# The last ten pairs of a convolution and two MLPs on one core, in an order of their own

## What is computed

```python
def _moe_ref(x, w_in, w_out):
    h = x @ w_in
    g = np.maximum(0.01 * h, h)
    return g @ w_out

def _moe2_ref(x, w_in, w_out, a, b):
    h = x @ w_in
    h2 = h * h
    h3 = h2 * h
    P = a[0] + a[1] * h + a[2] * h2 + a[3] * h3
    Q = 1.0 + np.abs(b[0]) * np.abs(h) + np.abs(b[1]) * h2
    g = P / (Q + 1e-06)
    return g @ w_out
```

## Time and profile before

| | us |
|---|---|
| median of 3 runs | 1347.91 (1347.9 to 1348.41) |
| the profiled execution | 1347.41 |
| its span, first to last instruction | 1345.5 |
| busy in the span: TensorE | 1264.7 (94%) |
| VectorE | 1059.5 (79%) |
| ScalarE | 1033.0 (77%) |
| GpSimd | 618.7 (46%) |

### The profile page before, as it was taken

The page is one execution under the profiler, slowest core; times in us unless marked ns, Lnnn a source line. Parts: engine busy times, 40 slices in busy tenths (PEclk is TensorE's granted clock), DMA queues, the critical chain, the costliest instruction groups (busy, mean ns, idle before and its releaser), DMA issues.

```text
span 1345.5 us, 14840 instructions
## 1 busy us (share of the span) xinstructions
PE 1264.7 (94%) x5724; PEld 1027.6 (76%) x5724; DVE 1059.5 (79%) x945; ACT 1033.0 (77%) x1027; POOL 618.7 (46%) x265
## 2 busy tenths in 40 slices
PE   7989999999999999999999999999999999999774
PEld 6768787877878787787877878787787878778553
DVE  3667878878788788878878787877878788787896
ACT  4677777878777877887877877787787788788763
POOL 0034454544545445445445454454544544545664
PEclk8999999999999999999999999999999999999887
DMA  6200000000000000000000000000000000000000
GB/s 191 78 1 13 0 25 1 12 13 1 24 1 25 0 12 13 1 25 0 13 13 13 13 0 25 1 12 14 12 13 1 25 1 13 1 1 12 0 12 12
DMA packets 25093, 21.74 MB, mean 16 GB/s; under 512 B 2909, under 2 KB 23997, under 8 KB 25023
## 3 DMA queue, kind: packets, MB, share of 16 engines
q1 hardware_dynamic: 25023, 20.80, 5.3%
...
## 4 chain that ended last, share of the span: by engine, by line
PE 58%; DVE 20%; ACT 11%; POOL 5%; issue 4%; DMA 1%; POOLq 0%; SPq 0%; DVEq 0%; ACTq 0%
PE h L611 29%; DVE den L508 6%; PE acc L621 5%; PE acc L630 5%; PE acc L631 5%; PE acc L623 5%; PE acc L622 5%; DVE hi L496 5%; DVE den L502 5%; POOL den L313 4%; ACT rec L394 4%; ACT rec L397 2%; ACT hi L389 2%; ACT h L385 2%; PE h L576 2%
## 5 line engine op out<-in xcount | busy, mean ns | idle before, releaser
L313 POOL TENSOR_TENSOR den<-den,rec 128x1024 f32<-128x1024 f32 x128 | 313.2, 2447 | 706.3 <-DVE den L508 415.6
L611 PE MATMUL h<-xs,wa 128*128 128x512 f32 x2520 | 612.5, 395 | 25.3 <-DVE xs L475 15.0
L611 PEld LDWEIGHTS h<-xs,wa 128*128 128x128 f32 x2520 | 471.5, 189 | 145.5 <-DVE xs L475 19.9
L319 POOL TENSOR_TENSOR lo<-den,rec 128x1024 fp32r<-128x1024 f32 x128 | 308.6, 2411 | 11.0 <-DVE den L508 11.0
L496 DVE SCALAR_TENSOR_TENSOR hi<-pol,coef_a,rec 128x1024 fp32r<-128x1024 f32 x128 | 164.3, 1283 | 94.6 <-issue 48.3
L621 PE MATMUL acc<-hi,wb 128*128 128x512 f32 x512 | 206.4, 403 | 20.0 <-DVE xs L489 19.9
L522 DVE TENSOR_TENSOR lo<-h,hi 128x1024 fp32r<-128x1024 f32 x128 | 156.3, 1221 | 86.8 <-ACT hi L389 86.8
L630 PE MATMUL acc<-lo,wb 128*128 128x512 f32 x512 | 201.5, 394 | 20.1 <-POOL lo L319 20.1
L363 ACT ACTIVATE rec<-h 128x1024 f32<-128x1024 f32 x124 | 127.3, 1027 | 111.6 <-PE h L611 111.6
L385 ACT ACTIVATE h<-h 128x1024 f32<-128x1024 f32 x128 | 129.3, 1010 | 98.6 <-PE h L611 98.6
L623 PE MATMUL acc<-hi,wb 128*128 128x512 f32 x512 | 201.0, 393 | 0.0
...
## 6 DMA issues: line engine op xcount, KB each, us to landing
...
```

The lines of the kernel that those rows point to most:

```text
L313: nc.gpsimd.tensor_tensor(den[k][:, :], den[k][:, :], rec[n % RECS][:, :], ALU.mult).then_inc(s_den, 1)
L319: nc.gpsimd.tensor_tensor(lo2[k][:, :], den[k][:, :], rec[(n - 1) % RECS][:, :], ALU.mult).then_inc(s_lo2, 1)
L611: last = T.matmul(dst[:, half, :], lhs, xs[m][:, part, :], start=(j == 0), stop=(j == 4))
```

## The change

Pairs 118 to 127 get a function of their own, `tail(n)`, on TensorE, ScalarE, VectorE and GpSimd; the steps before them stay as they were. In it:
- the hidden tiles go through three PSUM tensors by a table, `tail_ps`: 118 `h2`, 119 `h1`, 120 `acc0`, 121 `h2`, 122 `h1`, 123 `acc0`, 124 `h1`, 125 `acc0`, 126 `h2`, 127 `h1`;
- the third power of the polynomial is written in place in PSUM (`pol_3_all`), and `quotient_hi` and `residue` read it there. A hidden tile is therefore in use until the residue, where before it was free after the polynomial, and the up matmuls of a later pair wait for `s_res` instead of `s_pol`;
- the denominator has three buffers, `den0`, `pol1` and `den1`, and the polynomial's first power only `pol0`;
- ScalarE does the reciprocal of pair n-1 behind the first three instructions of pair n, VectorE the quotient of pair n-1 behind the polynomial of pair n, GpSimd the low part of pair n-2 behind the denominator of pair n, and TensorE the down matmuls of pair n-3 behind the up matmuls of pair n (`LAG2_TAIL = 3`);
- block 14 leaves at n = 123 (moves) and 124 (transposes into `h2`, copies); the last block's transposes go into `acc0`.

```diff
+LAG2_TAIL = 3
+TAIL_FOLD, TAIL_OUT, TAIL_END = 5, 6, 3
...
+    TAIL = PAIRS - LEAD
...
+        tail_ps = (h2, h1, acc[0], h2, h1, acc[0], h1, acc[0], h2, h1)
+
         def hidden_2(n):
 
-            if n > PAIRS - LEAD and n % 2:
-                return acc[0] if n > PAIRS - STEPS else h1
-            return h2
+            return tail_ps[n - TAIL] if n >= TAIL else h2
+
+        def den_of(n):
+
+            return (den[0], pol[1], den[1])[(n - TAIL) % 3] if n >= TAIL else den[n % 2]
+
+        def pol_of(n):
+
+            return pol[0] if n >= TAIL else pol[n % 2]
+
+        def pol_3_all(n):
+
+            return hidden_2_all(n) if n >= TAIL else pol[n % 2][:, :]
...
+            # GpSimd
+            def tail(n):
+                if n < PAIRS:
+                    denominator(n)
+                if n == TAIL:
+                    quotient_lo(TAIL - 1)
+                if TAIL <= n - 2 < PAIRS:
+                    quotient_lo(n - 2)
...
+            # ScalarE
+            def tail(n):
+                if n == TAIL + 1:
+                    split_x2(BLOCKS - 1)
+                if n < PAIRS:
+                    absolute(n)
+                    slope(n)
+                    first_power(n)
+                if n == TAIL + TAIL_FOLD:
+                    out_leaves(BLOCKS - 2)
+                if n == TAIL + TAIL_OUT:
+                    out_copies(BLOCKS - 2)
+                if TAIL <= n - 1 < PAIRS:
+                    reciprocal(n - 1)
+                if n == PAIRS + TAIL_END:
+                    out_leaves(BLOCKS - 1)
+                    out_copies(BLOCKS - 1)
...
             # VectorE
             def quotient_hi(n):
...
-                V.scalar_tensor_tensor(hi2[k][:, :], pol[k][:, :], coef_a[:, 0:1], rec[n % RECS][:, :],
+                V.scalar_tensor_tensor(hi2[k][:, :], pol_3_all(n), coef_a[:, 0:1], rec[n % RECS][:, :],
...
-                V.scalar_tensor_tensor(pol[k][:, :], pol[k][:, :], coef_a[:, 1:2], hidden_2_all(n),
+                V.scalar_tensor_tensor(pol_3_all(n), pol_of(n)[:, :], coef_a[:, 1:2], hidden_2_all(n),
...
+            def tail(n):
+                if n == TAIL + 1:
+                    split_x2(BLOCKS - 1)
+                if n == TAIL + TAIL_OUT:
+                    out_sums(BLOCKS - 2)
+                if n < PAIRS:
+                    polynomial(n)
+                if n == TAIL + TAIL_FOLD:
+                    out_moves(BLOCKS - 2)
+                if TAIL <= n - 1 < PAIRS:
+                    quotient_hi(n - 1)
+                    product(n - 1)
+                    residue(n - 1)
...
+            # TensorE
+            def tail(n):
+                c = BLOCKS - 1
+                if n == TAIL + TAIL_OUT:
+                    pe.wait_ge(s_res, n - 2)
+                    transpose_out(c - 1)
+                if n < PAIRS:
+                    if n == TAIL:
+                        pe.wait_ge(s_pol, n)
+                    elif n == TAIL + 1:
+                        pe.wait_ge(s_lo1, PAIRS)
+                    elif n == TAIL + 2:
+                        pe.wait_ge(s_x2_lo, 2 * c + 1)
+                    elif n == TAIL + 8:
+                        pe.wait_ge(s_ot_sum, 2 * c)
+                    else:
+                        pe.wait_ge(s_res, n - 1 if n > TAIL + 5 and n < TAIL + 8 else n - 2)
...
+                    up(1, n, hidden_2(n), x2_rest_ready, s_h2)
+                k0 = n - LAG2 if n < TAIL + LAG2 else n - LAG2_TAIL
+                if n != TAIL + LAG2 and k0 < PAIRS:
...
+                    pe.wait_ge(s_hi2, k0 + 1)
+                    down(1, k0, hi2[k], lo2[k], lambda: pe.wait_ge(s_lo2, k0 + 1), s_acc2)
```

More of the change, by code:

```diff
@@ L187, in runs, with every_step @@
             return 0 <= index < count
-        def every_step(step):
-            for n in range(-LEAD, PAIRS + OUT_AT + 1):
+        def every_step(step, tail):
+            for n in range(-LEAD, TAIL):
                 step(n)
+            for n in range(TAIL, PAIRS + TAIL_END + 1):
+                tail(n)
         order = [0, 1, 4, 2, 3, 5, 6, 7] + list(range(PIECES, 2 * PIECES))
@@ L345, in _, with absolute, slope, first_power @@
             nc.scalar.preload_act_table(ACT.Abs_reciprocal_sqrt)
+            def absolute(n):
+                if n == 0:
+                    act.wait_ge(s_coef, 2)
+                    act.wait_ge(s_wlo, 2 * PIECES)
+                act.wait_ge(s_h2, n + 1)
+                wait(act, s_lo2, n + 1 - RECS)
+                nc.scalar.activation(rec[n % RECS][:, :], hidden_2_all(n), ACT.Abs).then_inc(s_abs, 1)
+            def slope(n):
+                act.wait_ge(s_abs, n + 1)
+                if n == TAIL + 1:
+                    act.wait_ge(s_res, TAIL)
+                else:
+                    wait(act, s_lo2, n - 2 if n > TAIL + 2 else TAIL if n == TAIL + 2 else n - 1)
+                nc.scalar.activation(den_of(n)[:, :], rec[n % RECS][:, :], ACT.Identity, scale=coef_b[:, 1:2],
+                                     bias=coef_b[:, 0:1]).then_inc(s_slope, 1)
+            def first_power(n):
+                if n > TAIL:
+                    act.wait_ge(s_pol, n)
+                wait(act, s_res, min(n, TAIL) - 1)
+                nc.scalar.activation(pol_of(n)[:, :], hidden_2_all(n), ACT.Identity, scale=coef_a[:, 3:4],
+                                     bias=coef_a[:, 2:3]).then_inc(s_lin, 1)
+            def reciprocal(n):
+                r = rec[n % RECS][:, :]
+                act.wait_ge(s_den, n + 1)
+                nc.scalar.activation(r, den_of(n)[:, :], ACT.Abs_reciprocal_sqrt,
+                                     bias=one[:, 0:1]).then_inc(s_rsq, 1)
+                act.wait_ge(s_rsq, n + 1)
+                nc.scalar.activation(r, r, ACT.Square).then_inc(s_rec, 1)
+            def split_x2(c):
+                act.wait_ge(s_acc1, STEPS * c + STEPS)
+                wait(act, s_h2, STEPS * c)
+                nc.scalar.activation(xs[1][:, 0:3:2, :], acc[0][:, :, :], ACT.Copy).then_inc(s_x2_hi, 1)
+            def out_copies(c):
+                act.wait_ge(s_ot, c + 1)
+                wait(act, s_stored, 16 * c)
+                for half in range(2):
+                    nc.scalar.activation(out_tok[:, 2 * half:2 * half + 2, :], out_half(c, half)[:, :, 0:D],
+                                         ACT.Copy).then_inc(s_ot_copy, 1)
             def step(n):
@@ L366, in step @@
                 if phase == OUT_AT and runs(o0, BLOCKS):
[L367 to L376 removed]
+                    out_copies(o0)
@@ L398, in step @@
+                act.wait_ge(s_lky, m0 + 1)
+                wait(act, s_acc1, m0 - 1)
+                nc.scalar.activation(hi1[m0 % 2][:, :], hidden_1_all(n), ACT.Copy).then_inc(s_hi1, 1)
+                for j in range(*split_with(m0)):
+                    split_hi(j)
+                if n >= 0:
+                    reciprocal(n)
                 if phase == FOLD_AT and runs(o0, BLOCKS):
                     out_leaves(o0)
+            def tail(n):
+                if n == TAIL + 1:
+                    split_x2(BLOCKS - 1)
+                if n < PAIRS:
+                    absolute(n)
+                    slope(n)
+                    first_power(n)
+                if n == TAIL + TAIL_FOLD:
[7 more added lines that the diff above has]
+                    out_copies(BLOCKS - 1)
@@ L416, in _ @@
             split_hi(2)
-            every_step(step)
+            every_step(step, tail)
         @block.vector
@@ L533, in out_sums @@
                     rest = out_tok[:, 2 * half:2 * half + 2, P:D]
-                    V.tensor_tensor(rest, out_half(half)[:, :, D:2 * P], rest, ALU.add).then_inc(s_ot_sum, 1)
+                    V.tensor_tensor(rest, out_half(c, half)[:, :, D:2 * P], rest, ALU.add).then_inc(s_ot_sum, 1)
             def step(n):
```

122 lines of the change are left out of this document (50 added, 72 removed).

## The result

| | before | after |
|---|---|---|
| median, us | 1348.11 (4 runs, 1347.9 to 1348.41) | 1358.96 (4 runs, 1357.86 to 1360.31) |
| profiled span, us | 1345.5 | 1357.1 |

The changed kernel takes 1.0081 of the time before, with a 95% interval of 1.0063 to 1.0098: slower by 11 us.

What follows compares the result with a forecast made beforehand. The tail, through VectorE and GpSimd, was taken to bound the kernel. Long waits of 18.8 us less a gain of 8.4 gave +10.4, so 1358.3 us; 8 in 10 within 1352.5 to 1362.5.

Steps and rivals of the forecast that it cites:

- What it removes: Tail: VectorE no longer collides with GpSimd on SBUF ports (12 us); a late pair costs 7.14 us instead of 8.36.
- the ring: Late tail: loop of absolute, slope, denominator and low part through rec and GpSimd, 7.14 us per pair.
- Pair 118: Tail start: reciprocal now behind ScalarE's split and three instructions of the next pair; residue 118 ends 6.3 us late.
- Pairs 120 to 122: Up of 121 waits for residue 118, down of 120 for the move-out of acc1; residue 122 ends 3.3 us late.
- Pairs 123 and 124: Ups of 124 and 125 wait for residues 122 and 123: steps of 13.3 and 14.4 us, residue 124 14.3 late.
- The end: Pairs 125 to 127: two loops of 7.14, then 4.9 us with product blocked 1.0; residue 127 ends 10.4 late.
- three rings: Long waits at pairs 122 to 124, adding 5.3 + 6.2 + 7.3 = 18.8 us over steps of 7.14.
- The closing stretch: From the last residue to the span's end: 11.45 us, the same work in both kernels, so 0 change.
- A: Rival: the tail's rings don't close, only the 7.14 us loop is left, a gain, 1339.5 us; 4%.
- B: Rival: TensorE's three bursts after gaps of 6 to 9 us run at 2.4 GHz, 5 us less, 1353.3; 12%.
- C: Rival: PSUM operands don't free the port, pairs step at 8.36 as before, 1366 us; 6%.
- D: Rival: overlapping handovers make the waits cost less than half, within 0.2% of before, 1348 us; 5%.

Runs made afterwards that it cites:

- e10: e5 with the polynomial kept in SBUF instead of in place in PSUM; 1348.52 us, 1.0009 of before.
- e5: Changed kernel with the one-pair lag undone, down matmuls two pairs behind and block 14's sums moved out at n = 121; 1337.34 us, 0.9929 of before.
- e4: Changed kernel with the polynomial kept in SBUF and a new third denominator buffer; 1367.83 us, 1.0153 of before.
- e7: e3 with a fourth buffer for rec, so absolute of pair n waits for the low part of n-4; 1338.24 us, 0.9928 of before.
- e1: Changed kernel with block 14's sums moved out of acc1 ahead of pair 123's polynomial and ScalarE instructions; 1353.94 us, 1.0046 of before.
- e2: Changed kernel with h2, h1, acc0 used in turn and block 14 transposed into h1 at n = 128; 1344.26 us, 0.9974 of before.
- e6: Changed kernel with 16 unread matmuls added before the up of 125, where TensorE was idle; 1355.58 us, 1.0060 of before.
- e0: The changed kernel run again, unedited, as yardstick; 1358.83 us, 1.0085 of before.
- e3: Changed kernel with the edits of e1 and e2 together; 1340.70 us, 0.9950 of before.

## Why the prediction was right

**What it removes.** Right. The place of the polynomial was the cause of the blocked time (e10 against e5: 11 us; e4, with a wait of its own in it: 9), and all residues fell to 1.28 us. The section on the cores says that the engines meet only at semaphores; VectorE and GpSimd meet here as well. The estimate of the ring, 7.14, stands at 7.1 to 7.4, and e7 shows that it is the ring by opening it. VectorE's own work for a pair, taken as 6.35, is 6.22 there.

**Pair 118.** Laid out as 6.3 us late. After the 1.07 us by which this execution's tail begins later, its residue ends 6.2 late (1264.60 against 1257.30). e5, without the lag, has it on time. The path is told wrongly, though: the terms written down reach 1259.4 and not 1259.7, and the last wait was another.

```profile
1259.34 1.06 ACT L400 ACTIVATE rec<-rec 128x1024 f32<-128x1024 f32 x1
...
1259.55 1.29 DVE L577 SCALAR_TENSOR_TENSOR h<-pol,coef_a,h 128x1024 f32<-128x1024 f32 x1
1260.75 1.28 DVE L557 SCALAR_TENSOR_TENSOR hi<-h,coef_a,rec 128x1024 fp32r<-128x1024 f32 x1
```

The reciprocal of 118 (L400) was done at 1260.40, and `quotient_hi` began at 1260.75 (less the 1.07, the forecast's 1259.7), right behind the polynomial of 119 (L577), which stands ahead of it on VectorE.

**Pairs 120 to 122.** The up of 121 waited 5.6 us (laid out: 6), and its ten matmuls took 4.6 (4.4). The down of 120 waited 8.7 and the step to residue 122 was 12.3 (12.4). e1, which moves only the move-out, takes 3.7 of it away; 1.5 over the ring of 7.14 are left there, and `quotient_hi` still waits 1.37 us for the down matmuls.

**Pairs 123 and 124.** 13.4 and 14.5 (13.3 and 14.4); e2, which changes only the tiles and where block 14 is transposed, removes both. The slow up matmuls of 125 are a term of their own, 2 us by e6. Less 7.14 each, the three long steps measured 5.2, 6.2 and 7.3, together 18.7, where the sum had 18.8. The path inside the last two is again not quite the one told. The reciprocals of 123 and 124 were done at 1307.53 and 1322.20, and their `quotient_hi` began at 1308.09 and 1322.55, behind the polynomials of 124 and 125. The "reciprocal 2.3, handover 0.5" of the sum has the right length for this other path.

**The end.** 127's residue 10.6 late after taking off the 1.07 (10.4), `product` blocked for 1.0 us as laid out.

**Where it was loose.** The sum named three rings as if they were independent of the lag. They are not: e5 keeps the tile table and has none of them. The lag makes a tile's life a pair longer, and only then is a table that gives pairs 124 and 125 the tile of two pairs before too tight. Either edit takes the loss away: another table with the late transposes (e2), or no lag with the early move-out (e5). The closing stretch, taken as 11.45 in both, is 11.4 in the changed kernel's profile, but 10.8 in e0's. And the up of 124 was taken at the full clock; e0 shows that after its gap of 3.2 us it can be slow as well, 2 us more. That the forecast lies within 0.7 us of the median is therefore in part luck; the mechanism and the steps are not.

**The rivals.** A (no ring closes) was not this kernel. Its time, 1339.5, is near that of e3, 1340.7, in part by chance: e3's steps of 122 to 124 are still 3.0 us over three of 7.14, and its closing stretch is 1.5 shorter. B (high clock), C (the port not freed) and D (half the waits) didn't occur; C's kernel is about that of e4, which took 1367.8 where C had 1366. The Trainium skill's rule in "SBUF — State Buffer", section "SBUF: two separate sides", by which a VectorE instruction with two SBUF inputs takes the ports that GpSimd needs, agrees with all traces: in the tail no VectorE instruction with an input in PSUM took over 1.4 us in any run. The fixed cost for PSUM operands, left out of the sum against the Trainium skill's "VectorE: DVE Perf Modes", section on the TRN2 errata, did not show: `quotient_hi` and `residue` from PSUM took 1.28 us each.
